# Attention fused into two gated layers: pairing the query blocks as (1,2), (3,4), (5,6), (7,8) and scoring all of them with split products

## What is computed

```python
scores = q @ k.T / sqrt(64);  scores[block_i < block_j] = -1e9
attn   = exp(scores - rowmax); attn /= attn.sum(-1) + 1e-9
x = attn @ v                                      # (2304, 512)
h = x @ w_in;   x = (h * sigmoid(h)) @ w_out      # 512 -> 2048 -> 512
h = x @ w_in2;  x = (h * sigmoid(1.702 h)) @ w_out2
```

## Time and profile before

| | |
|---|---|
| Median of 3 runs | 949.5 us (949.18 to 950.19) |
| Profiled execution, its own time | 948.78 us |
| Its span, first to last instruction | 947.0 us |
| PE busy | 929.0 us, 98% |
| DVE, ACT, POOL busy | 527.8, 384.7, 299.4 us |
| Mean granted TensorE clock | 0.996 |

### The profile page before, as it was taken

One profiled execution on the slowest core, in us unless ns is written; L12 is line 12 of the kernel. 1 busy time (PEld: TensorE's weight loads), 2 busy tenths in 40 slices (PEclk: granted clock), 3 DMA queues, 4 the chain that ended last, 5 costly groups with the idle time before them and its releaser, 6 DMA issues.

```text
span 947.0 us, 14419 instructions
## 1 busy us (share of the span) xinstructions
PE 929.0 (98%) x5304; PEld 794.9 (84%) x5304; DVE 527.8 (56%) x1096; ACT 384.7 (41%) x854; POOL 299.4 (32%) x408
## 2 busy tenths in 40 slices
PE   5899999999999999999999999999999999999998
PEld 4788877787778777877788889999999999999997
DVE  6778656665656556755445435454654455644443
ACT  4677534453435344543323323232433233523222
POOL 5899437654544365435718100000000000000000
PEclk8999999999999999999999999999999999999999
DMA  8555695795688764888537976434363434363431
GB/s 248 172 162 150 185 321 161 232 322 198 207 278 257 255 195 126 266 275 268 189 106 283 380 298 210 123 112 127 107 188 112 133 102 133 105 196 104 130 101 67
DMA packets 65190, 179.57 MB, mean 190 GB/s; under 512 B 7136, under 2 KB 8800, under 8 KB 59232
## 3 DMA queue, kind: packets, MB, share of 16 engines
q1 hardware_dynamic: 64688, 177.99, 59.1%
q10 hardware_dynamic: 432, 0.66, 0.2%
HBM read 130.02 MB, written 44.56 MB: 184 GB/s over the span
## 4 chain that ended last, share of the span: by engine, by line
PE 94%; POOL 1%; DVE 1%; ACT 1%; issue 0%; POOLq 0%
PE ps_y L967 20%; PE ps_y L1025 13%; PE ps_a L1026 7%; PE ps_h L950 7%; PE ps_h L952 6%; PE ps_h L951 6%; PE ps_a L929 5%; PE ps_a L917 4%; PE ps_a L998 4%; PE ps_a L1001 4%; PE ps_a L1000 4%; PE ps_h L998 3%; PE ps_h L1001 3%; PE ps_h L1000 3%; PE ps_a L869 2%; PE ps_a L897 2%
## 5 line engine op out<-in xcount | busy, mean ns | idle before, releaser
L967 PE MATMUL ps_y<-g_hi,w_hl 128*128 128x512 f32 (+1 forms) x640 | 189.2, 378 | 0.0
L1025 PE MATMUL ps_y<-o_hi,w_out 128*128 128x512 f32 x368 | 139.9, 391 | 0.0
L967 PEld LDWEIGHTS ps_y<-g_hi,w_hl 128*128 128x128 f32 x640 | 112.0, 189 | 16.6 <-DVE g_lo L1376 0.4
L967 PE MATMUL ps_y<-g_lo,w_hl 128*128 128x512 f32 (+1 forms) x320 | 118.5, 370 | 0.0
L1152 ACT ACTIVATE g_f<-ps_h 128x512 f32<-128x512 f32 (+1 forms) x71 | 40.9, 576 | 188.7 <-PE ps_h L952 188.6
L950 PE MATMUL ps_h<-x_hi,w_hl 128*128 128x512 f32 (+1 forms) x284 | 111.6, 393 | 1.1 <-POOL w_hl L750 1.1
L1371 DVE SCALAR_TENSOR_TENSOR g_f<-g_f,ps_h 128x512 f32<-128x512 f32 x63 | 43.3, 687 | 119.1 <-ACT g_f L1152 118.8
L952 PE MATMUL ps_h<-x_lo,w_hl 128*128 128x512 f32 (+1 forms) x284 | 107.7, 379 | 0.0
L951 PE MATMUL ps_h<-x_hi,w_hl 128*128 128x512 f32 (+1 forms) x284 | 107.2, 377 | 0.0
L1026 PE MATMUL ps_a<-o_hi,w_out 128*128 128x256 f32 x368 | 103.0, 280 | 0.0
L1133 ACT ACTIVATE p_sb<-ps_a,nmax 128x512 f32<-128x512 f32 (+4 forms) x128 | 72.4, 573 | 68.4 <-DVE nmax L1340 68.0
(11 more groups left out here) (151 smaller groups left out, 1899.7 us busy)
## 6 DMA issues: line engine op xcount, KB each, us to landing
w_form<-f_split SPq DMA_DIRECT2D x168, 256.0 KB, 2.7
w_hl<-w_split SPq DMA_DIRECT2D x30, 1024.0 KB, 7.5
w_raw<-w_chunks SPq DMA_DIRECT2D x42, 512.0 KB, 5.2
w_split<-w_hl SPq DMA_DIRECT2D x16, 1024.0 KB, 7.8
f_split<-stage SPq DMA_DIRECT2D x24, 512.0 KB, 5.8
o_split<-stage SPq DMA_DIRECT2D x16, 512.0 KB, 4.3
w_out<-o_split SPq DMA_DIRECT2D x16, 512.0 KB, 7.1
k_raw<-kT SPq DMA_DIRECT2D x28, 288.0 KB, 5.8
```

What stands on the lines that cost most here:

```text
L967: last = nc.tensor.matmul(bank_y(t, k), lhs, rhs, start=(part == 0 and f == 0 and (t > 0 or k % 2 == 0)), stop=(part == 2 and f == NF - 1) ...
L1025: nc.tensor.matmul(y_main(k), lhs, rhs[:, h, 0:512], start=begin, stop=end, skip_group_check=True)
```

## The change

Query blocks 1 to 8 become four pairs, (1,2), (3,4), (5,6), (7,8), with widths of 192, 320, 448 and 576 keys. Each of the eight rows is one pair of one head; all rows of head 0 come ahead of those of head 1. All are scored by the two split products; the row of 576 as two halves of 288 in two banks. For jobs 0 to 3 the scores rotate through three banks and transposes and values have the spare bank of `ps_y` alone; later jobs score in banks 0 and 1 and put the row of 192 behind the second half of the wide one. `ends`, `q_end` and `queries_end` are gone. The keys of head 1 are stored backwards by blocks, so that the last key blocks of all pairs form four 64x64 products of probabilities and values at the end of `values`. The splitting of keys and queries, and the copy of the high keys by DMA, are done head by head. All places are set anew.

```diff
-WIDTH = (576, 128, 512, 512, 384, 384, 256, 256)
-QCOL = (448, 0, 320, 320, 192, 192, 64, 64)
+HEAD = (0, 0, 0, 0, 1, 1, 1, 1)
+PAIR = ((3, 1, 2, 0, 3, 1, 2, 0), (3, 0, 2, 1, 3, 0, 2, 1))
+BANKS = ((((0, -2), (1, -1)), ((2, 0),), ((0, 1),), ((1, 1),), ((1, 4), (2, 2)), ((0, 3),), ((1, 5),), ((2, 5),)),
+         (((0, -1), (1, 0)), ((1, None),), ((0, 1),), ((1, 2),), ((0, 3), (1, 4)), ((1, None),), ((0, 5),), ((1, 6),)))
-NORMED = (1, 3, 4, 5, 8, 8)
+NORMED = ((1, 4, 5, 6, 8, 8), (1, 3, 5, 7, 8, 8))
-START_AT = (-8, 19, 49, 75, 106)
+START_AT = (-6, 22, 50, 78, 106)
-UNIT_AT = ((0, 5, 11, 15), (0, 7, 13, 19))
-BATCH_AT = ((12, 13, 16, 21, 27, 29), (9, 13, 18, 20, 27, 30))
-PV_AT = (33, 32)
+UNIT_AT = ((0, 4, 8, 12), (-1, 4, 7, 15))
+SECOND_AFTER = (1, 0)
+BATCH_AT = ((8, 12, 18, 22, 26, 28), (7, 13, 19, 24, 27, 30))
+PV_AT = (34, 34)
-MAX_AFTER = (0, 2)
-EXP_AFTER = ((1, 1), (2, 2))
-MULTIPLY_AFTER = ((4, 4), (5, 7))
+MAX_AFTER = (1, 2)
+EXP_AFTER = ((1, 2), (2, 2))
+MULTIPLY_AFTER = ((5, 6), (3, 5))
-PREP_AT = ((-12, -11, -7, -5, -7, -3, 0, -5, -5), (-12, -12, -9, -6, -6, -5, -4, -7, -9))
+PREP_AT = ((-23, -16, -13, -8, -11, 2, -17, -2, -8, 3), (-16, -9, -14, -7, -11, -4, -11, -5, -13, -8))
...
+def width(p):
+    return BLK * (2 * p + 3)
...
             def load_keys(n):
                 if n >= 2:
                     sp.wait_ge(s_kl, 2 * before(n) + 2)
...
-                    sp.wait_ge(s_sc, ROWS * before(n) + 2)
...
-            def copy_keys(n):
-                sp.wait_ge(s_kh, 2 * (n + 1))
-                sp.dma_start(k_mask[0:D, :, :].bitcast(F32), k_both[0:D, :, :].bitcast(F32)).then_inc(s_kc, 16)
+            def copy_keys(n, h):
+                sp.wait_ge(s_kh, 2 * n + h + 1)
+                sp.dma_start(k_mask[0:D, h, :].bitcast(F32), k_both[0:D, h, :].bitcast(F32)).then_inc(s_kc[h], 16)
             def place_masks():
-                sp.wait_ge(s_mask, 8)
+                sp.wait_ge(s_mask, 2 + 3 * NPAIR)
...
-                    if place in PREP[7]:
-                        keys_low(PREP[7][place], 0)
-                        keys_low(PREP[7][place], 1)
+                    for h in range(2):
+                        if place in PREP[6 + h]:
+                            keys_low(PREP[6 + h][place], h)
...
+            def scores(n, u, i):
+                h = HEAD[UNITS[u][0]]
+                if u % 2 == 0 and i == 0:
+                    pe.wait_ge(s_ql, 2 * n + h + 1)
+                    pe.wait_ge(s_kl, 2 * n + h + 1)
+                    if n < FIRST:
+                        pe.wait_ge(s_km, 2 * n + h + 1)
+                    else:
+                        pe.wait_ge(s_kc[h], 16 * (n - FIRST + 1))
+                    if n == 0 and u == 0:
+                        pe.wait_ge(s_maskd, 64)
+                r = UNITS[u][i]
+                p = pair(n, r)
+                q = slice(P * p, P * p + P)
+                banks = BANKS[late(n)][r]
+                w = width(p) // len(banks)
+                for j, (b, taken) in enumerate(banks):
+                    dst = bank(b)[:, 0:w] if len(banks) == 2 else scored(n, r)
+                    a = (S - width(p)) * h + w * j
+                    if taken is not None and ROWS * n + taken > 0:
+                        pe.wait_ge(s_ex, ROWS * n + taken)
...
+                    nc.tensor.matmul(dst, q_twice[:, h, q], k_both[:, h, a:a + w], start=True, stop=False,
+                                     skip_group_check=True)
+                    last = nc.tensor.matmul(dst, q_mask[:, h, q], k_mask[:, h, a:a + w], start=False, stop=True,
+                                            skip_group_check=True)
                 last.then_inc(s_sc, 1)
...
-                for t in range(NJ):
+                for t in range(NPAIR):
                     for h in range(2):
                         d = slice(D * h, D * h + D)
-                        last = nc.tensor.matmul(bank(2)[d, OFF[t]:SQ], v_sb[:, n % 2, t, d], pt_sb[:, h, t, OFF[t]:SQ],
-                                                start=(t == 0), stop=(t == NJ - 1), skip_group_check=True)
+                        i = 2 * NPAIR - 1 - t if h else t
+                        nc.tensor.matmul(lane(n)[d, P * t:SQ], v_sb[:, n % 2, i % NPAIR, d], pt_sb[:, i, P * t:SQ],
+                                         start=(t == 0), stop=False, skip_group_check=True)
+                for p in range(NPAIR):
+                    for h in range(2):
+                        d = slice(D * h, D * h + D)
+                        q = P * p + BLK
+                        last = nc.tensor.matmul(lane(n)[d, q:q + BLK], v_half[d, n % 2, p, :], pt_half[d, p, :],
+                                                start=False, stop=(p == NPAIR - 1), skip_group_check=True)
...
             def keys_high(n, h):
                 loaded(act, s_k, n)
                 if n:
-                    act.wait_ge(s_sc, ROWS * n)
+                    act.wait_ge(s_sc, ROWS * (n - 1) + scored_by(h))
```

More of the change, by code:

```diff
@@ L217, in build @@
         over = ExitStack()
-        mask_q = sb(over, "mask_q", [P, SQ - 2 * BLK])
-        mask_k = sb(over, "mask_k", [P, S])
+        mask_q = sb(over, "mask_q", [P, SQ])
+        mask_k = sb(over, "mask_k", [P, 2, S])
         e_nmax = sb(over, "e_nmax", [P, JOBS])
@@ L320, in build @@
         s_kl = sem("s_kl")
-        s_qe = sem("s_qe")
-        s_kc = sem("s_kc")
+        s_kc = [sem(f"s_kc{h}") for h in range(2)]
         s_km = sem("s_km")
@@ L404, in pieces, with lane, scored, probs @@
-        def pieces(n, b):
+        def lane(n):
+            return ps_y[:, 1536:2048] if n < FIRST else bank(2)
+        def scored(n, r):
+            banks, p = BANKS[late(n)][r], pair(n, r)
+            b = banks[0][0]
+            if len(banks) == 2:
+                return ps_a[:, 512 * b:512 * (b + 2)].rearrange("p (b c) -> p b c", b=2)[:, :, 0:S // 2]
+            a = 0 if banks[0][1] is not None else S // 2
+            return bank(b)[:, a:a + width(p)]
+        def probs(n, r):
+            a, p = P_AT[HEAD[r]][pair(n, r)], pair(n, r)
+            return p_sb[:, a:a + width(p)]
@@ new lines, in block_of_keys, with half_tile, whole_tile @@
+        def block_of_keys(h, b):
+            a = BLK * (NQ - 1 - b) if h else BLK * b
+            return slice(a, a + BLK)
+        def half_tile(p):
+            a = P_AT[0][p] + P * (p + 1)
+            return p_sb[:, a:a + P]
+        def whole_tile(h, p, t):
+            a = P_AT[h][p] + P * t + BLK * h
+            return p_sb[:, a:a + P]
+        def pieces(n, b):
+            whole, halves = BATCHES[late(n)][b]
+            flat = lane(n)
+            if halves:
+                return [(pt_half[:, :, :], flat.rearrange("p (m c) -> p m c", c=P)[:, :, BLK:P])]
+            p = whole[0][1]
+            if len(whole) == 2 and whole[1][1] == p:
+                both = pt_sb[:, :, P * p:P * p + P].rearrange("p (a t) c -> p a t c", t=p + 1)
+                return [(both[:, 0::2 * NPAIR // (p + 1) - 1, :, :], flat.rearrange("p (h t c) -> p h t c", h=2, c=P))]
+            views = []
@@ L406, in pieces @@
             col = 0
[L407 to L410, removed]
+            for h, p in whole:
+                a, w = (2 * NPAIR - 1 - p) * h, P * (p + 1)
+                views.append((pt_sb[:, a:a + p + 1, P * p:P * p + P],
+                              flat[:, col:col + w].rearrange("p (t c) -> p t c", c=P)))
                 col += w
[L412 to L421, removed]
@@ L908, in transposes @@
                 else:
-                    before = b - 2 if n < FIRST else b - 1
-                    if before >= 0:
-                        pe.wait_ge(s_ta if by_act(n, before) else s_td, takes(n, before))
-                col = 0
-                for rows, t0, t1 in BATCHES[b]:
-                    for r in rows:
-                        for t in range(t0, t1):
-                            a = P_AT[r] + P * t
-                            last = nc.tensor.transpose(lane(n, b)[:, col:col + P], p_sb[:, a:a + P], ident[:, :])
-                            col += P
+                    pe.wait_ge(s_ta if by_act(n, b - 1) else s_td, takes(n, b - 1))
+                whole, halves = BATCHES[late(n)][b]
+                tiles = [whole_tile(h, p, t) for h, p in whole for t in range(p + 1)] + [half_tile(p) for p in halves]
+                for i, tile in enumerate(tiles):
+                    last = nc.tensor.transpose(lane(n)[:, P * i:P * i + P], tile, ident[:, :])
                 last.then_inc(s_tr, 1)
@@ L1058, in _ @@
                     place = STEP * c + i
-                    if place in UNIT:
-                        unit(*UNIT[place])
+                    for row in range(2):
+                        if place in ROW[row]:
+                            scores(*ROW[row][place], row)
                     if place in BATCH:
@@ L1206, in _ @@
             early_exp(1)
-            queries_end(0)
             queries_high(0, 0)
```

201 lines of the change are left out of this document (84 added, 117 removed).

## The result

The changed kernel takes 951.4 us in the median of 20 runs (950.7 to 952.8), the kernel before 949.5 (948.8 to 950.2). The ratio is 1.0021, 95% interval 1.0015 to 1.0027: slower by 1.9 us, where I had forecast 944.5. The profiled execution of the changed kernel took 952.12 us. First the page's head: the span is 3.3 us longer than the earlier trace rows, though TensorE is busy slightly less than the 929.0 us of before.

What follows compares the result with a forecast made beforehand. PE was taken to bound late jobs, PE and POOL nearly evenly tile 0. Late jobs 5.3 less 0.6 for unit 2's waits, plus 0.3 in tile 0, gave 5.0 us: 944.5 us median, 8-in-10 range 940.5 to 953.

Steps and rivals of the forecast that it cites:

- the sum for tile 0 and jobs 0 to 3: Tile 0: 1.8 + 1.1 - 1.0 - 0.6 - 1.0 = 0.3 us gained, bounds 3.0 gained to 3 lost.
- Rival C: Tile 0 comes out 3 us worse than summed, through ACT's blocks on loads and exponentials: 947.5 us; chance 0.13.
- Job 4's queries and POOL's wait, charged 1.0: End of tile 0: queries wanted seven places earlier, POOL waits for job 4's first keys ahead of chunk 14; 1.0 us lost.
- PE saves 4 x 0.44 = 1.8: Jobs 0 to 3 in tile 0: each saves PE the same 0.44 us as a late job, 1.8 us.
- Keys of job 1 ahead of the exponential, charged 0.6: Job 0: ACT meets job 1's key load ahead of row 3's exponential, on which unit 2 waits; 0.6 to 1 us lost.
- The 3.2 us of waits stay in sum.: Tile 0: PE's waits for exponentials keep their 3.2 us total, although three score banks let unit 1 start earlier.
- Scores, gain 0.54 a job: Each job's scores: 2.90 us of new split products replace 3.44, taking 0.11 us per product of 192 columns.
- Rival A: Scores: each fp32r product of 192 columns costs 0.32 us instead of 0.11, 13.4 us more, 957.9 us; chance 0.14.
- Values, loss 0.10 a job: Each job's values: the same work by columns, plus one more change of the array's shape costing 0.10 us.
- Job gain 0.44: PE work per job falls by 0.54 - 0.10 = 0.44 us; twelve late jobs give 5.3 us if PE never waits.
- Rival B: Late jobs: unit 2 waits a whole instruction, 0.4 us, in each; 0.8 us gained in all, 948.7 us; chance 0.11.
- The signs that I named: Chunk 15 begins between 101.7 and 105.5; POOL's wait near 2 us; tile 0 shift above 3 us means wrong.

Runs made afterwards that it cites:

- experiment 3: Changed kernel with ACT's high keys of job 1, head 0, one place later, behind the exponential of job 0's row 3: 951.6 us, 1.0028 of the kernel before.
- experiment 5: Changed kernel with job 4's keys split at their old places and its queries and keys loaded at places 74 and 73: 948.5 us, 0.9998 of the kernel before.
- Version 10: Changed kernel, job 4's loads early, its keys at old places, job 1's head 0 keys behind row 3's exponential, preparation of jobs 1 to 3 reordered: 947.0 us.
- experiments 2: Changed kernel with two idle F32 matmuls of 256 columns in PE's gap ahead of chunk 0, results thrown away: 950.9 us, 1.0016 of the kernel before.
- experiment 1: Kernel before, with `ends` of job 0 issued at place -6, outside PE's idle time, instead of -8: 950.8 us, 1.0016 of the kernel before.
- 6: Changed kernel with the edits of experiment 5 and experiment 3 together: 947.6 us, 0.9982 of the kernel before.
- 8: 7 with ACT's and DVE's preparation in jobs 1 to 3 reordered, so a gate and a transposes copy stand ahead: 947.0 us, 0.9975 of the kernel before.
- 7: 6 plus two idle F32 matmuls of 256 columns in PE's gap ahead of chunk 0: 947.8 us, 0.9983 of the kernel before.
- experiment 4: Changed kernel with the splitting and first DMA copy of job 4's keys at the old kernel's places: 951.5 us, 1.0025 of the kernel before.

## Why the prediction was wrong

**The failed step is the sum for tile 0 and jobs 0 to 3.** I had it 0.3 us better; in the profiled executions it is 6.6 us worse at chunk 15. In the medians it is less: 1.9 us and the late gain, which between chunk 15 and the second layer is 3.0 to 3.4 us in the traces of the changed kernel and experiments 3, 5 and 10, make about 5 us. Rival C had this sign and place at half the size, and my bound of 3 us from below failed. I took that bound from the longest waits of the old kernel, which a new order of the work doesn't keep. Term by term, of which the measured ones don't add up to the whole loss:

- *Job 4's queries and POOL's wait, charged 1.0.* They cost 2.2 to 2.9 us (experiment 5 against the change), the largest piece. I foresaw both waits and mis-priced them. POOL's wait was 5.0 us in the changed kernel's profile (96.18 - 4.98 = 91.2, when chunk 13 was done), but 2.7 and 2.6 in those of experiments 2 and 3, near the 2 us that I named, with ACT's wait at 2.4 and 2.7, and chunk 15 was as late. What I left out is that at place 92 ACT's wait has a copy of transposes behind it on which PE then stands for 2.8 to 3.4 us. I also credited 1.1 for POOL's keys lying in better gaps. The old wait at 41.04 did go, and one of 1.2 for chunk 14 came at 103.18, behind job 4's keys.
- *PE saves 4 x 0.44 = 1.8.* Wrong for job 0. `ends` there ran in PE's idle time ahead of `x_lo` and cost nothing; moving it onto the path costs 1.5 us, 0.7 to 2.4 (experiment 1). So unit 0's new scores replace nothing on the path.
- *Keys of job 1 ahead of the exponential, charged 0.6.* It is 0.67 us of ACT's time (26.07), and unit 2's wait is 0.3 to 0.5 us shorter without it (experiment 3). A price in the total is not shown: nothing in experiment 3, and in 6 against 5 a difference that only the slower half of experiment 5 has.
- *Masks and unit 0 of job 0, charged 1.0.* Nothing: unit 0 waits for nothing at 20.15.
- *"The 3.2 us of waits stay in sum."* The waits for exponentials did (2.6), but 3.0 for batches came on top. With the spare bank as the only lane, a batch needs the copy of the one before, and in jobs 1 and 3 that stands behind preparation in ACT's order. Reordering it is worth 0.6 us (10 against 6) or 0.7 (8 against 7).
- *What remains.* Version 10 is 2.3 us faster than before where the late jobs alone give 3.0 or more, so about 1 us of tile 0 is still lost (chunk 15 begins at 105.87, before at 104.50). Its trace has PE waits of 2.1 us for exponentials, 1.9 for `x_lo` and 1.2 for job 4's low keys, among others; which of them it is was not tried. Ahead of job 4's hold-ups a gain doesn't come through: experiments 2 and 3 showed 0.5 us or nothing.

**Scores, gain 0.54 a job.** Right: 3.44 became 1.06 + 0.81 + 0.59 and, with 192 at 0.09 and 0.12, 0.42 = 2.88, a gain of 0.56. Rival A (0.32 for 192 columns) is out. So is a floor of 0.107 us by the loading of the stationary side, which would follow from the Trainium skill's figure in "TensorE: Matmul & The Clock Gate", section "LDWEIGHTS (loading the stationary operand)": the first product of 192 columns takes 385.56 - 385.47 = 0.09. The measurement decides; 192 columns lie on the line of 0.43 ns a column.

**Values, loss 0.10 a job.** It was 2.92 - 2.74 = 0.18. By columns the sixteen small products are 512 x 0.83 ns = 0.42, and they take 0.62, so 0.20 comes on top where I had 0.10. Whether the second change of the array's shape costs it or the small products themselves was not tried.

**Job gain 0.44.** 0.30 in the job shown, as 31.02 - 30.72. The values took 0.08 of the difference. The rest, 0.44 - 0.08 - 0.30 = 0.06 and the 0.02 that the scores were better, I put down to the layer matmuls, which start later behind the new narrow products (375.60 to 375.86 is 0.26 where the same step was 0.23, 0.69 for three). Between chunk 15 and the second layer the jobs gave 3.3 us, forecast 5.3 less 0.6 for waits. Rival B is out: no late job waits, and the 0.6 charged for unit 2 was not due.

**The signs that I named** decided it at once: chunk 15 outside 101.7 to 105.5, POOL's wait 5.0 for 2, the shift at the end of tile 0 above 3 us. ACT's wait for job 4's queries, named at 2 to 3 us, is absent from the changed kernel's profile, where ACT came to them only at 97.30 and they had landed. It is 2.4, 2.7 and 3.4 us in experiments 2, 3 and 4, whose executions reach that place earlier.

## What to carry to other kernels

Where two engines run nearly even, as PE and POOL in tile 0 here, read for each moved step what the other engine's next step needs from it, and price the wait by the time between the two places in both walks, not by the waits of the old profile. Instructions that lie in an engine's idle time cost nothing, so look there before counting their removal as a gain. When an experiment that removes a wait shows nothing, look for a second wait where the engines meet again and remove both: experiment 4 gave nothing, experiment 5 gave 2.2 to 2.9 us. And before crediting a part of the work with lost or gained time, look at a second execution of the same instructions.

## What the chip showed beyond that

A matmul's clock differed between executions of one instruction sequence for some 4 us (up by 18.85 or from 22.8 us on), and chunk 2 began at 30.8 or 32.6 with it, while the medians of the two kernels are 0.6 us apart with a second edit between them. Between the changed kernel's profile and experiment 5's, chunk 2 moved by 3.1 us with the same instructions ahead of it. A single profile is a poor judge of a stretch that follows an idle TensorE. In the trace of the changed kernel the records of the clock begin only at 23.2 us, so the column of the granted clock reads 1.00 for the stretch before; the distance of starts, 0.24 us for 288 columns, tells the level.
